# Issuing the last three quad transfers of the down-projection weights earlier in SyncE's queue

## The chip, the cores and the metric

The kernel runs on one core of one Trainium2 chip. The metric is the device time of one execution in microseconds (us). Before the change it is 816.56 us, the median of three runs (816.48 to 816.95).

## What is computed

Three stages follow one another, for a batch of 4 and a sequence of 448 tokens: attention with 12 heads of 64 and a soft cap on the scores, a mixer with a 768x768 theta product, sines and cosines, and a 768x768 channel product, and a second mixer:

```python
def _moe2_ref(x, w_tok1, w_tok2, w_ch1, w_ch2):          # x: (4, 448, 768)
    xt = x.transpose(0, 2, 1)
    h = np.maximum(xt @ w_tok1, 0.0) @ w_tok2            # tokens: 448 -> 256 -> 448
    u = x + h.transpose(0, 2, 1)
    h2 = np.maximum(u @ w_ch1, 0.0) @ w_ch2              # channels: 768 -> 1536 -> 768
    return (u + h2).astype(np.float32)
```

The change touches only the stretch that computes `u @ w_ch1` for the first two of the four batch elements, and in it only the preparation of `w_ch2`.

## The kernel before

All large products are fp32. Each operand is split into a rounded part `hi` (ScalarE, ACT) and a remainder `lo` (VectorE, DVE), and TensorE (PE) makes three matmuls for each pair of tiles (L1716 to L1718: hi by hi, hi by lo, lo by hi).

The two channel products of the second mixer are done in two rounds (s = 0 and 1; two batch elements each) by a seven-product scheme of the Strassen kind on 2x2 blocks. The first product ("rise", `w_ch1`) has 6 groups g of 7 products, always in the order M1, M2, M6, M7, M4, M5, M3. The second ("fall", `w_ch2`) takes the same seven in the same order. Every product of the rise needs one weight part of 128x384 (192 KB); it is 9 matmuls on TensorE, three for each of three column blocks. M1, M2 and M4 use blocks of the weights as they are in memory; M6, M7, M5 and M3 use sums of blocks ("quads"), which are prepared once:

- SyncE (SP) loads four blocks, a quad buffer of 768 KB (`load_fall_quads`, DMA at L640);
- GpSimd (POOL) makes four 128x384 additions in place, one after the other (`sum_fall_quads` over `sum_quads`, L878, L880, L882, L884), each counted in `fall_quad_steps`;
- SP waits for all four and writes the buffer to a scratch in HBM (`store_fall_quads`, wait and DMA at L646 and L647).

There are six such pairs (0 to 5) for `w_ch2`. Pairs 0 to 2 are handled before the stretch of the change; pairs 3, 4 and 5 in it. The buffers are 1, 2 and again 1, so the load of pair 5 waits for the store of pair 3 (L639). Two things need all six stores: ScalarE's `copy_first` of group 5 of the first round (L1029 to L1033), which writes over one of the buffers, and the first load of a summed part in the fall (L654 to L656).

SP is the only issuer of DMAs in this stretch, and its program is one list: a wait in it holds back everything behind it. `load_product` (L621, DMA at L630) loads the weight part of one product into one of 7 slots, after the product that used the slot 7 products earlier was read by TensorE (`part_read`). ScalarE rounds a part (L1021) three products ahead of the one that it is otherwise serving; DVE makes its remainder (L1409) at the same lead; TensorE waits for the remainder (L1941) and starts the product. Both work in program order too:

```python
def rise(s, g, steps):                       # ScalarE, L1119
    for m in steps:
        round_part(part_of(s, g, m) + 3)
```

Below, "M6 of group 4" is the product (0, 4, M6), and its part, load, rounding and remainder go by the same name.

Of the kernel before, what the change touches and what calls it, by code (L numbers as in the profile page):

```python
# [63 lines left out]
M1, M2, M3, M4, M5, M6, M7 = range(1, 8)  # L64
# [33 lines left out]
def fall_quads_use(pair):  # L98

    return ((0, 1), (0, 2), (0, 3), (1, 1), (2, 1), (1, 2))[pair]  # L100
# [33 lines left out]
def mixer_kernel(nc, kq_t, v, cap, w_theta, w_tok_r_t, w_tok_i_t, w_ch, w_tok1, w_tok2,  # L134
# [3 lines left out]
    with ctx:  # L138
# [319 lines left out]
        def after(engine, semaphore, value):  # L458

            if value > 0:  # L460
                engine.wait_ge(semaphore, value)
# [27 lines left out]
        def _(sp):  # L489
# [131 lines left out]
            def load_product(s, g, m):  # L621

                q = part_of(s, g, m)
                after(sp, part_read, last_use(q))
                if m in QUADS:
                    sp.wait_ge(quads_stored, 16 * (g + 1))
                    weights = quad_scratch[g, QUADS[m]]
                else:
                    weights = w_ch1[g, int(m == M4), int(m != M1)]
                sp.dma_start(part_raw[SLOTS[q]][:, :], weights).then_inc(part_loaded[SLOTS[q]], 16)  # L630

            def load_fall_quads(pair):

                e, use = fall_quads_use(pair)
                if pair == 0:
                    sp.wait_ge(tok_split, 2)
                elif pair == 3:
                    sp.wait_ge(tok2_ready, D_TILES * BATCH)
                after(sp, fall_quads_stored[e], 16 * (use - 1))  # L639
                sp.dma_start(fall_quads[e][:, :, :], w_ch2[pair].rearrange("m k p n -> p (m k) n")  # L640
                             ).then_inc(fall_quads_loaded[e], 16)

            def store_fall_quads(pair):

                e = fall_quads_use(pair)[0]
                sp.wait_ge(fall_quad_steps, 4 * (pair + 1))  # L646
                sp.dma_start(fall_quad_scratch[pair].rearrange("q p n -> p q n"), fall_quads[e][:, :, :]  # L647
                             ).then_inc(fall_quads_stored[e], 16)

            def load_fall(s, m, pair, g_half):  # L650

                q, group = fall_part(s, m, pair, g_half), 2 * pair + g_half
                after(sp, part_read, last_use(q))
                if m in QUADS:  # L654
                    for e, uses_of_buffer in enumerate((3, 2, 1)):
                        sp.wait_ge(fall_quads_stored[e], 16 * uses_of_buffer)  # L656
                    weights = fall_quad_scratch[group, QUADS[m]]
                else:
                    weights = w_ch2[group, int(m == M4), int(m != M1)]
                sp.dma_start(part_raw[SLOTS[q]][:, :], weights).then_inc(part_loaded[SLOTS[q]], 16)  # L660
# [3 lines left out]
            def spill(b):  # L664

                sp.wait_ge(u2_made, D_TILES * (b + 1))
                sp.dma_start(spilled_rows[:, :, (b - 2) * SEQ:(b - 1) * SEQ], x_of(b)).then_inc(spilled, 16)
# [55 lines left out]
            def store_quarter(s, m, m_half, n):  # L723

                sp.wait_ge(fall_adds_made, fallen(s, m, D_PAIRS - 1))
                sp.dma_start(out_t[2 * s + n].rearrange("(d p) n -> p d n", p=P)[:, m_half:D_TILES:2, :],
                             x_t[:, 0, m_half:D_TILES:2, n * SEQ:(n + 1) * SEQ]).then_inc(out_stored, 16)
# [16 lines left out]
            def load_first_blocks():  # L744

                sp.wait_ge(spilled, 32)
                sp.wait_ge(part_read, fall_part(0, M1, D_PAIRS - 1, 1) + 1)
                for k in range(K_PAIRS):
                    load_block_tile(0, b12_raw[k], 2 * k, 1)
                for k in range(2):  # L750
                    load_block_tile(0, b22_raw[k], 2 * k + 1, 1)
                load_block(B11, block_raw[B11], 0)

            def load_second_blocks():

                sp.wait_ge(part_read, fall_part(0, M2, D_PAIRS - 1, 1) + 1)
                load_block_tile(1, b22_raw[2], 5, 1)
                for k in range(K_PAIRS):
                    load_block_tile(1, b11_raw[k], 2 * k, 0)
                load_block(B21, block_raw[B21], 0)  # L760

            def reload_x(piece):

                n, d0 = piece // 2, 3 * (piece % 2)
                sp.wait_ge(out_stored, 64)
                sp.dma_start(x_t[:, 0, d0:d0 + 3, n * SEQ:(n + 1) * SEQ],
                             spilled_rows[:, d0:d0 + 3, n * SEQ:(n + 1) * SEQ]).then_inc(x_reloaded, 16)

            for s in range(ROUNDS):
                for g in range(0 if s else 2, C_PAIRS):  # L770
                    for m in M_ORDER:
                        load_product(s, g, m)
                        if (s, g, m) == (0, 2, M2):
                            spill(3)
                        elif (s, g, m) == (0, 2, M4):
                            store_fall_quads(3)
                        elif (s, g, m) == (0, 3, M1):
                            load_fall_quads(4)
                        elif (s, g, m) == (0, 3, M3):
                            store_fall_quads(4)  # L780
                        elif (s, g, m) == (0, 4, M2):
                            load_fall_quads(5)
                        elif (s, g, m) == (0, 5, M1):
                            store_fall_quads(5)
                        if (s, g, m) == (1, 0, M4):
                            store_quarter(0, M5, 1, 1)
                        if (s, g, m) == (1, 1, M2):
                            store_quarter(0, M3, 0, 1)
                    if s == 1 and 1 <= g <= 4:
                        reload_x(g - 1)  # L790
                for m in M_ORDER:
                    for pair in range(D_PAIRS):
                        for g_half in range(2):
                            load_fall(s, m, pair, g_half)
                            if (s, m, pair, g_half) == (0, M6, 1, 0):
                                load_first_blocks()
                            if (s, m, pair, g_half) == (0, M7, 1, 0):
                                load_second_blocks()
                            if (m, pair, g_half) == (M7, 0, 1):
                                store_quarter(s, M2, 0, 0)  # L800
                            if (m, pair, g_half) == (M3, 0, 1):
                                store_quarter(s, M4, 1, 0)
# [1268 lines left out]
```

## Time and profile before

| what | value |
|---|---|
| median of three runs | 816.56 us |
| the profiled execution's own time | 816.48 us |
| its span, first to last instruction | 814.3 us |
| TensorE busy | 805.9 us (99%) |
| VectorE busy | 660.1 us (81%) |
| ScalarE busy | 456.6 us (56%) |
| GpSimd busy | 147.4 us (18%) |
| granted TensorE clock, mean | 1.000 |

Times in the profile count from the span's start. The stretch of the change reaches from about 524 us (M7 of group 2) to about 558 us (M1 of group 5). SPq is the row of SyncE's own DMA issues: its start is when the issue began, so a late start there is a wait in SP's program. A DMA's landing is when the last of its sixteen completions arrived.

### The profile page before, as it was taken

The numbers are of one execution on the slowest core, as the hardware profiler recorded it, in microseconds if no ns is written. First come the engines' busy times: TensorE is split into PE (matmuls) and PEld (weight loads), VectorE is DVE, ScalarE is ACT, GpSimd is POOL, SyncE is SP. The second block draws the span as 40 slices with busy tenths as digits, with TensorE's granted clock in tenths as the row PEclk, the third lists the DMA queues.
The fourth block names the chain that finished last, engine by engine and source line by source line (L and its number), as shares of the span: only waits on it lengthen the run. The fifth ranks groups of instructions, "written<-read, shape, count | busy, mean of one in ns | idle before, by whom it ended". The sixth has DMA issues, their size and how long they took to land.

```text
span 814.3 us, 13137 instructions
## 1 busy us (share of the span) xinstructions
PE 805.9 (99%) x4852; PEld 693.7 (85%) x4852; DVE 660.1 (81%) x1060; ACT 456.6 (56%) x687; POOL 147.4 (18%) x108
## 2 busy tenths in 40 slices
PE   9999999999999999999999999999999999999998
PEld 6555555579999999999999999999998889999997
DVE  5899999989967676866566679887979998789884
ACT  6999999947655454822114116344655645457551
POOL 0254566332000000014442320222000000000000
PEclk9999999999999999999999999999999999999999
DMA  6557765444421221325667655665375455543443
GB/s 175 159 143 171 188 164 134 111 107 106 100 75 43 67 67 49 117 88 178 214 212 253 195 151 185 236 217 178 107 254 164 140 175 175 147 137 109 146 121 127
DMA packets 103295, 119.79 MB, mean 147 GB/s; under 512 B 38880, under 2 KB 100928, under 8 KB 103232
## 3 DMA queue, kind: packets, MB, share of 16 engines
q1 hardware_dynamic: 103008, 118.73, 49.7%
q8 instruction: 39, 0.64, 0.4%
q10 hardware_dynamic: 224, 0.23, 0.1%
q14 instruction: 24, 0.20, 0.1%
HBM read 89.96 MB, written 28.96 MB: 146 GB/s over the span
## 4 chain that ended last, share of the span: by engine, by line
PE 83%; DVE 10%; issue 4%; ACT 2%; DMA 1%; SPq 0%; POOL 0%; DVEq 0%; POOLq 0%; ACTq 0%
PE psum L1718 23%; PE psum L1716 23%; PE psum L1717 23%; PE psum L1772 6%; PE psum L1728 4%; PE psum L1799 2%; DVE part_lo L1409 1%; DVE seven_lo L1459 1%; DVE tile_sums L1186 1%; PE psum L1730 1%; DVE block_lo L1401 1%; ACT ring L919 1%; DMA part_raw<-fall_quad_scratch 1%; PE psum L1807 1%; ACT ring L922 1%
## 5 line engine op out<-in xcount | busy, mean ns | idle before, releaser
L1021 ACT ACTIVATE part_hi<-part_raw 128x384 fp32r<-128x384 f32 x168 | 83.9, 516 | 65.2 <-DMA part_raw<-fall_quad_scratch 35.9
L1409 DVE TENSOR_TENSOR part_lo<-part_raw,part_hi 128x384 fp32r<-128x384 f32 x168 | 96.7, 577 | 22.3 <-ACT part_hi L1021 22.2
L1716 PE MATMUL psum<-seven_hi,part_hi 128*128 128x448 f32 x252 | 91.9, 365 | 1.5 <-DVE seven_lo L1459 0.7
L1716 PE MATMUL psum<-block_hi,part_hi 128*128 128x448 f32 x252 | 91.2, 362 | 0.7 <-DVE part_lo L1409 0.7
L1717 PE MATMUL psum<-block_lo,part_hi 128*128 128x448 f32 x252 | 91.4, 363 | 0.0
L1718 PE MATMUL psum<-seven_hi,part_lo 128*128 128x448 f32 x252 | 91.4, 363 | 0.0
L1718 PE MATMUL psum<-block_hi,part_lo 128*128 128x448 f32 x252 | 91.2, 362 | 0.0
L1717 PE MATMUL psum<-seven_lo,part_hi 128*128 128x448 f32 x252 | 91.2, 362 | 0.0
L1772 PE MATMUL psum<-ring,values 128*32 128x448 f32 x768 | 81.4, 542 | 0.3 <-issue 0.3
L919 ACT ACTIVATE ring<-psum,score_scale 128x1344 f32<-128x1344 f32 (+1 forms) x48 | 75.3, 1568 | 8.7 <-PE psum L1730 5.6
L922 ACT ACTIVATE ring<-ring,cap_col 128x1344 f32<-128x1344 f32 (+1 forms) x48 | 77.2, 1608 | 1.6
L1772 PEld LDWEIGHTS psum<-ring,values 128*32 128x32 f32 x768 | 22.8, 109 | 42.8 <-issue 42.8
L1039 ACT ACTIVATE h_raw<-h_raw 128x448 f32<-128x448 f32 x48 | 27.7, 577 | 56.3 <-DVE h_raw L1421 32.4
L1716 PE MATMUL psum<-theta_hi,x_hi 128*128 128x384 f32 x168 | 56.4, 335 | 0.0
L1717 PE MATMUL psum<-theta_lo,x_hi 128*128 128x384 f32 x168 | 56.1, 334 | 0.0
L1718 PE MATMUL psum<-theta_hi,x_lo 128*128 128x384 f32 x168 | 56.1, 334 | 0.0
L1716 PEld LDWEIGHTS psum<-seven_hi,part_hi 128*128 128x128 f32 x252 | 47.2, 187 | 7.4 <-issue 2.0
L1718 PE MATMUL psum<-u_hi,channel_lo 128*128 128x448 f32 x144 | 52.3, 363 | 0.0
L1718 PE MATMUL psum<-token_hi,z_lo 128*128 128x448 f32 x144 | 52.3, 363 | 0.0
L1717 PE MATMUL psum<-u_lo,channel_hi 128*128 128x448 f32 x144 | 52.2, 362 | 0.0
L1717 PE MATMUL psum<-token_lo,z_hi 128*128 128x448 f32 x144 | 52.2, 362 | 0.0
L1716 PE MATMUL psum<-token_hi,z_hi 128*128 128x448 f32 x144 | 51.8, 360 | 0.0
(184 smaller groups left out, 2165.2 us busy)
## 6 DMA issues: line engine op xcount, KB each, us to landing
part_raw<-moe_w_ch SPq DMA_DIRECT2D x72, 192.0 KB, 2.4
kq_raw<-kq_t SPq DMA_DIRECT2D x47, 224.0 KB, 3.9
part_raw<-quad_scratch SPq DMA_DIRECT2D x48, 192.0 KB, 2.4
part_raw<-fall_quad_scratch SPq DMA_DIRECT2D x48, 192.0 KB, 2.4
values<-v SPq DMA_DIRECT2D x48, 112.0 KB, 3.5
inverse_rows<-inverse_scratch SPq DMA_DIRECT2D x12, 448.0 KB, 6.2
rows_scratch<-turned SPq DMA_DIRECT2D x112, 48.0 KB, 1.7
x_rows<-rows_scratch SPq DMA_DIRECT2D x28, 192.0 KB, 2.4
```

The lines of the kernel that those rows point to most:

```text
L919: act.activation(places, psum[:, first:end, 0:SEQ], ACT.Tanh, scale=score_scale[:, :]).then_inc(tanh_done, 1)
L922: act.activation(places, places, ACT.Exp, scale=cap_col[:, :]).then_inc(probs_ready, 1)
L1021: act.activation(part_hi[SLOTS[q]][:, :], part_raw[SLOTS[q]][:, :], ACT.Copy).then_inc(part_hi_made, 1)
L1039: act.activation(h_raw[tile][:, :], h_raw[tile][:, :], ACT.Relu).then_inc(relu_made, 1)
L1186: dve.tensor_tensor(total, tiles_of_both(pair, A0, B0), tiles_of_both(pair, A1, B1), ALU.add).then_inc(tiles_added, 1)
L1409: dve.tensor_tensor(part_lo[slot][:, :], part_raw[slot][:, :], part_hi[slot][:, :].bitcast(F32), ALU.subtract).then_inc(part_lo_made, 1)
L1716: pe.matmul(out, left[0], right[0], start=start, stop=False)
L1717: pe.matmul(out, left[0], right[1], start=False, stop=False)
L1718: return pe.matmul(out, left[1], right[0], start=False, stop=stop)
L1728: b_mm = pe.matmul(psum[:, b_tile, 0:SEQ], left[s][b_rows, b_keys], right[s][b_rows, queries], start=step == 0, stop=step == 2 and b_tile ...
L1772: mm = pe.matmul(psum[rows, VALUES_BANK, 0:SEQ], own[:, block, 32 * h:32 * h + 32], ring[:, ring_place(pair, tile), :], start=n == 0, stop ...
L1799: mm = pe.matmul(psum[32 * n:32 * n + 32, SUMS_BANK, 0:SEQ], weights[:, :], moving, start=True, stop=True)
```

## The change

SP's list in the first round is rearranged; nothing else is touched, and every DMA and wait is still there once.

| step | before: behind the load of | after: behind the load of |
|---|---|---|
| store of pair 3 | M4, group 2 | M7, group 2 |
| load of pair 4 | M1, group 3 | M3, group 2 |
| store of pair 4 | M3, group 3 | M6, group 3 |
| load of pair 5 | M2, group 4 | M4, group 3 |
| store of pair 5 | M1, group 5 | M2, group 4 |

```diff
                         load_product(s, g, m)
                         if (s, g, m) == (0, 2, M2):
                             spill(3)
-                        elif (s, g, m) == (0, 2, M4):
+                        elif (s, g, m) == (0, 2, M7):
                             store_fall_quads(3)
-                        elif (s, g, m) == (0, 3, M1):
+                        elif (s, g, m) == (0, 2, M3):
                             load_fall_quads(4)
-                        elif (s, g, m) == (0, 3, M3):
+                        elif (s, g, m) == (0, 3, M6):
                             store_fall_quads(4)
+                        elif (s, g, m) == (0, 3, M4):
+                            load_fall_quads(5)
                         elif (s, g, m) == (0, 4, M2):
-                            load_fall_quads(5)
-                        elif (s, g, m) == (0, 5, M1):
                             store_fall_quads(5)
```

## Rows read from the trace of the kernel before

**Rows 1.** The page: busy us of each engine, share of the span, instructions

```profile
PE 805.9 (99%) x4852; PEld 693.7 (85%) x4852; DVE 660.1 (81%) x1060; ACT 456.6 (56%) x687; POOL 147.4 (18%) x108
```

**Rows 2.** Two stretches: us, busy (count) of PE, PEld, DVE, ACT, POOL, clock, DMA

```profile
530.00:543.00 13.00, 13.00 (x67) 12.19 (x66) 11.47 (x20) 6.48 (x14) 4.88 (x4) 1.00 0.58 189
543.00:557.00 14.00, 14.00 (x72) 13.13 (x71) 11.94 (x21) 6.29 (x13) 4.38 (x5) 1.00 0.73 226
```

**Rows 3.** SP's waits for POOL, 515 to 575: total us, times, longest

```profile
SPq L647 <- POOL fall_quads L884: 1.4, 3, 0.6
```

**Rows 4.** SP's issues in order of time: start, us, line, transfer

```profile
526.70 0.37 SPq L647 DMA_DIRECT2D fall_quad_scratch<-fall_quads  x1
...
529.58 0.32 SPq L630 DMA_DIRECT2D part_raw<-quad_scratch  x1
...
531.76 1.69 SPq L640 DMA_DIRECT2D fall_quads<-moe_w_ch  x1
...
543.07 0.37 SPq L647 DMA_DIRECT2D fall_quad_scratch<-fall_quads  x1
...
546.16 0.49 SPq L640 DMA_DIRECT2D fall_quads<-moe_w_ch  x1
...
557.39 0.37 SPq L647 DMA_DIRECT2D fall_quad_scratch<-fall_quads  x1
558.38 0.33 SPq L630 DMA_DIRECT2D part_raw<-moe_w_ch  x1
```

**Rows 5.** Issue to landing, us: issues at 516.03, 516.50, 546.16, 543.07, 557.39, 558.38, 426.03; median

```profile
fall_quads<-moe_w_ch SPq DMA_DIRECT2D x1, 768.0 KB, 5.8
part_raw<-quad_scratch SPq DMA_DIRECT2D x1, 192.0 KB, 5.8
fall_quads<-moe_w_ch SPq DMA_DIRECT2D x1, 768.0 KB, 6.2
fall_quad_scratch<-fall_quads SPq DMA_DIRECT2D x1, 768.0 KB, 4.2
fall_quad_scratch<-fall_quads SPq DMA_DIRECT2D x1, 768.0 KB, 4.1
part_raw<-moe_w_ch SPq DMA_DIRECT2D x1, 192.0 KB, 3.5
fall_quad_scratch<-fall_quads SPq DMA_DIRECT2D x1, 768.0 KB, 8.0
part_raw<-quad_scratch SPq DMA_DIRECT2D x48, 192.0 KB, 2.4
```

**Rows 6.** SP's issues around the one of 426.03

```profile
425.61 0.38 SPq L613 DMA_DIRECT2D quads<-moe_w_ch  x1
...
427.72 3.76 SPq L674 DMA_DIRECT2D block_scratch<-block_turned  x4
```

**Rows 7.** POOL's first addition of pairs 4 and 5; ns min/median/max of all six

```profile
537.89 1.40 POOL L878 TENSOR_TENSOR fall_quads<-fall_quads 128x384 f32<-128x384 f32 x1 [11.21 <-DMA fall_quads<-moe_w_ch]
...
552.42 1.27 POOL L878 TENSOR_TENSOR fall_quads<-fall_quads 128x384 f32<-128x384 f32 x1 [9.38 <-DMA fall_quads<-moe_w_ch]
...
L878 POOL TENSOR_TENSOR fall_quads<-fall_quads x6: 1013/1022/1404, 418.4 to 552.4; 128x384 f32<-128x384 f32 x6
```

**Rows 8.** One part from landing (516.50 + 5.8) to remainder: ACT, then DVE

```profile
522.30 0.53 ACT L1021 ACTIVATE part_hi<-part_raw 128x384 fp32r<-128x384 f32 x1 [2.09 <-DMA part_raw<-quad_scratch]
522.86 0.56 DVE L1409 TENSOR_TENSOR part_lo<-part_raw,part_hi 128x384 fp32r<-128x384 f32 x1 [0.86 <-ACT part_hi L1021]
```

**Rows 9.** First matmuls of M7 and M5 of group 3 and M6 of group 4

```profile
547.38 0.36 PE L1716 MATMUL psum<-block_hi,part_hi 128*128 128x448 f32 x1
550.99 0.36 PE L1716 MATMUL psum<-block_hi,part_hi 128*128 128x448 f32 x1
558.18 0.36 PE L1716 MATMUL psum<-block_hi,part_hi 128*128 128x448 f32 x1
```

**Rows 10.** ScalarE's `copy_first` of group 5, the first to need all six stores

```profile
569.18 0.55 ACT L1032 ACTIVATE h_raw<-psum 128x448 f32<-128x448 f32 x1 [1.95 <-PE psum L1718]
```

## The prediction

> **What bounds the kernel.** I read the engines' shares first, then stretches, then SP's issues, and at last single parts. TensorE is busy for 99% of the span [rows 1], and in the two stretches that hold nearly all of the change it is busy all the time, 13.00 of 13.00 us and 14.00 of 14.00, at a granted clock of 1.00, its level of 2.4 GHz [rows 2]. So no wait of TensorE exists here that an earlier transfer could remove. A product is nine matmuls, and its part's load falls due every 1.8 us: M7 and M5 of group 3 start at 547.38 and 550.99, two products apart, and from M5 to M6 of group 4, four products, it is 7.19 [rows 9].
>
> A part's load waits until TensorE has freed a slot, so the loads go out at the products' pace. For POOL, at the quad stores, SP waits only 1.4 us in three waits [rows 3]: the stores now stand where POOL has just finished; the load of pair 4 is issued at 531.76 and its store at 543.07, 11.3 us later; for pair 5 it is 546.16 and 557.39, 11.2 us [rows 4]. The change shortens the list between load and store: for pair 4 from six part loads (M2 to M3 of group 3) to three (M1, M2, M6), for pair 5 from six to four (M5, M3 of group 3, M1, M2 of group 4). At 1.8 us each that is 5.4 and 7.2 us instead of 10.8, while load, landing and four additions need about 11. The wait at the store must grow, and behind it on SP's queue stand the loads of parts.
>
> **What can be won.** Nothing that I can find. The last store is issued at 557.39 and lands 4.1 us later, at 561.5 [rows 4, 5]. The first instruction that needs it starts at 569.18, and it waited for TensorE [rows 10]. The store is 7.7 us early already. No instruction is removed or added, so the sum has only waits in it.
>
> **Step 1, the store of pair 3.** Before it is issued at 526.70, after a short wait for POOL [rows 3, 4]. It can't go earlier, as its additions are where they were. M4 of group 2, which stood in front of it, now goes behind: 1.1 us later, and landing behind the store. TensorE wants M4 only four products after M1 of that group; ScalarE rounds it after its copy of M1. I cost it at nothing; the cover is the seven slots. Without that cover it would be those 1.1 us.
>
> **Step 2, load and store of pair 4.** The load goes out behind M3 of group 2 (529.58, 0.32) at 529.95, 1.8 us earlier. Loads of this kind take 5.8 and 6.2 us to land [rows 5]; with 6.0 it is 535.95. From POOL's first addition to the store's issue it was 543.07 - 537.89 = 5.18 us for pair 4 and 557.39 - 552.42 = 4.97 for pair 5 [rows 4, 7]; I take 5.05, so the store goes out at 541.0. M6 of group 3, the part in front of it, is issued near 535.0 (1.8 us per part from 529.58). SP then stands for 5.7 us. Queued behind it are M7 (due 536.8), M4 (538.6) and M5 (540.4). An issue takes about 0.4 us with its gap, so M7 goes at 541.4, M4 at 541.8, the load of pair 5 at 542.2, then M5 and M3.
>
> When does M7 land? A part that was issued 0.47 us behind a quad load took 5.8 us: it landed 0.5 us after that load (522.3 against 521.8). One issued 0.99 us behind a store took 3.5: 561.9 against the store's 561.5 [rows 4, 5]. So a small load behind a large transfer lands about 0.45 us after it; the stores took 4.1 and 4.2 [rows 5]: M7 at 541.0 + 4.15 + 0.45 = 545.6. From landing to the remainder it is 522.30 to 523.42, 1.1 us [rows 8]; with 0.1 for TensorE's start, 1.2. M7 is ready at 546.8, and TensorE wants it at 547.38 [rows 9]. It holds by 0.6 us.
>
> Here a rule of the Trainium skill bears, and it speaks against the change. "DMA: Bandwidth & Descriptors", section "Queues, rings and completion order", says that on each DMA engine descriptors are consumed in ring order and that the completion is counted only after all earlier writes of that engine. The two rows on parts behind a large transfer agree. If instead a part landed on its own after 2.4 us, the median of these loads in the profile's page [rows 5], all of the late parts here would be in time and the sum would be nothing.
>
> **Step 3, load and store of pair 5.** Its buffer is free (the store of pair 3 landed near 531). Its load at 542.2 stands behind 768 KB of store and two parts. Alone such loads took 5.8 and 6.2; in the thickest queue of the trace a quad transfer took 8.0 [rows 5]. I take 6.3, nearest to the load of 546.16, which also had a store and parts ahead of it: landing 548.5. M5 of group 3, right behind, lands at 549.0 and is ready at 550.2; TensorE wants it at 550.99 [rows 9]: 0.8 us of spare. POOL needs 5.05 us again: store at 553.55, against 557.39. But M2 of group 4 is in front of it, issued at 545.8: SP stands for 7.4 us. M6 of group 4 was due at 547.6 and now goes at 554.0. It lands behind the store, 553.55 + 4.15 + 0.45 = 558.15, and is ready 1.2 us later, at 559.35. TensorE wants it at 558.18 [rows 9]. **TensorE idles 1.2 us before M6 of group 4.**
>
> The parts behind it land about 0.45 us apart, while TensorE takes 1.8 for each, so no second wait follows. The waits for M7 and M5 of group 3, if they come, don't add to this one: the time of M6 hangs on SP and POOL, not on TensorE. After it every load waits for TensorE's reading again and all of the rest shifts by the same amount, as TensorE is the bound (99%).
>
> **Sum.** The profiled execution took 816.48 us (span 814.3), 0.08 below the median. 816.48 + 1.2 = 817.7; on the median's footing 817.8, or 0.15% more.
>
> **Bounds of the unknown terms.** Short end: loads 5.8 and 5.8, additions 4 x 1.02 us, the median of the first of them [rows 7], and 0.1 between two, 4.4 in all. Then the store of pair 4 goes at 540.15, the load of pair 5 at 541.35, the second store at 551.55; M6 is ready 4.15 + 0.45 + 1.2 = 5.8 us later, at 557.35: no idle time. Long end: additions of 5.2 and a load of pair 5 in 8.0 us: first store at 541.15, load at 542.35, second store at 555.55, M6 ready at 561.35, 3.2 us idle; if the second store took 8.0 us too, 7.0. I take the middle, because the nearest rows in time, kind and queue are those of pairs 4 and 5.
>
> **Rivals.**
> - *The cover just holds* (22%). M6 of group 4 comes within some 0.3 us of its time. For it: the waits of 0.6 and 0.8 us that remain at M7 and M5, and that the additions on POOL are short where DVE is idle. Against: DVE is busy for 11.94 of 14.00 us there [rows 2], and the additions of pairs 4 and 5 began with 1.40 and 1.27 us in place of 1.02 [rows 7]. Time 816.5.
> - *The queue backs up* (27%), the rival on the slower side. Its place is the burst after SP's first stand: store, two parts, load, two parts, 2.3 MB within 2.5 us. Price: each us that the load of pair 5 lands later than 548.5 is one us of idle TensorE; it decides from about 549.0 on, where the total passes 0.2%. For it: the 8.0 us row. Against: that row had another 768 KB right ahead and four more stores behind it [rows 6]. With 8.0 us the idle time is 1.2 + 1.7 = 2.9, 819.5; with M5 and M3 of group 3 late too it is still 2.9.
> - *Faster* (4%): the additions leave the stretch from 552 to 557, and DVE's remainders there run alone. But TensorE waits for none of them [rows 2]. At most some tenths: 816.2.
>
> The forecast itself has 47%, a quarter of it or less (10%) above 1.63 us.
>
> **How the numbers follow.** 0.2% is 1.63 us and about what can be told from no change. Slower: 27 + 10 = 37%. Within 0.2%: 37 + 22 = 59%. Faster: 4%. The range goes from the case without a wait, 816.5, less the run's noise, to somewhat over 3.2 us of idle time (816.56 + 3.2 = 819.8): 816.4 to 819.9. The 7.0 us are outside, as the second store has no large transfer right ahead of it.
>
> **What would show it.** SP's issues: stores of pairs 4 and 5 at about 541.0 and 553.6, SP waiting at L647 for POOL some 5.7 and 7.4 us instead of under 1; M6 of group 4 issued at about 554.0; ScalarE idle before its rounding, ended by a DMA; one gap of TensorE near 558, ended by DVE's L1409. Wrong would be: no gap (then a landing or an addition is shorter than here), a gap at 547 or 551 (then the queue behind the first store is slower), or any gain.

## The result, and the profile after

The changed kernel takes 820.19 us (median of five runs, 818.53 to 822.99) against 816.48 for the kernel before (814.87 to 816.95). The ratio is 1.0057, 95% interval 1.0033 to 1.0082: slower, by 3.7 us. Two later comparisons of the same two kernels gave 819.50 against 816.07 (1.0036, 1.0013 to 1.0059) and 819.77 against 816.54 (1.0039, 1.0019 to 1.0059). The prediction was 817.8, with a range up to 819.9; the first median lies just above that range, the two later ones inside it. The direction and the place were right; the size was not.

The profiled execution took 819.77 us, with a span of 817.6 against 814.3. First the page's shares, then the two stretches of [rows 2] and the one behind them (columns as there):

```profile
PE 806.3 (99%) x4852; PEld 690.0 (84%) x4852; DVE 663.0 (81%) x1060; ACT 456.8 (56%) x687; POOL 145.0 (18%) x108
```

```profile
530.00:543.00 13.00, 13.00 (x67) 12.19 (x66) 12.38 (x20) 6.09 (x13) 4.79 (x4) 1.00 0.54 174
543.00:557.00 14.00, 12.42 (x61) 10.65 (x60) 9.21 (x16) 4.82 (x10) 4.66 (x4) 1.00 0.63 210
557.00:570.00 13.00, 11.83 (x59) 10.78 (x58) 10.45 (x22) 6.66 (x14) 0.00 (x0) 1.00 0.64 200
```

The shares say nothing: TensorE is "99%" busy in both. The stretches do. From 543 to 557 TensorE was busy for 14.00 of 14.00 us and now is for 12.42, and behind 557 it is idle for 1.17 more. Its clock is granted in full (1.00). The cause is one row of SP's waits, 515 to 575, where [rows 3] had 1.4 us:

```profile
SPq L647 <- POOL fall_quads L884: 18.5, 3, 8.4
```

SP's issues, to be read beside [rows 4]: the three quad stores (L647), the two quad loads (L640), and the parts (L630) behind them.

```profile
527.62 0.37 SPq L647 DMA_DIRECT2D fall_quad_scratch<-fall_quads  x1
...
530.24 0.51 SPq L640 DMA_DIRECT2D fall_quads<-moe_w_ch  x1
...
534.88 0.33 SPq L630 DMA_DIRECT2D part_raw<-quad_scratch  x1
542.18 0.38 SPq L647 DMA_DIRECT2D fall_quad_scratch<-fall_quads  x1
542.66 0.44 SPq L630 DMA_DIRECT2D part_raw<-quad_scratch  x1
543.46 0.69 SPq L630 DMA_DIRECT2D part_raw<-moe_w_ch  x1
544.20 0.56 SPq L640 DMA_DIRECT2D fall_quads<-moe_w_ch  x1
...
555.63 0.38 SPq L647 DMA_DIRECT2D fall_quad_scratch<-fall_quads  x1
556.11 1.72 SPq L630 DMA_DIRECT2D part_raw<-quad_scratch  x1
```

M6 of group 3 goes out at 534.88, and then SP issues nothing for 6.9 us, until POOL is done. The store of pair 5 is issued at 555.63, 1.8 us earlier than before, but SP had stood before it for 8.4 us, with M6 of group 4 next in its list. How long the quad loads of 530.24 and 544.20, the store of 555.63 and the part of 556.11 took to land (last number), as in [rows 5]:

```profile
fall_quads<-moe_w_ch SPq DMA_DIRECT2D x1, 768.0 KB, 6.8
fall_quads<-moe_w_ch SPq DMA_DIRECT2D x1, 768.0 KB, 6.4
fall_quad_scratch<-fall_quads SPq DMA_DIRECT2D x1, 768.0 KB, 4.4
part_raw<-quad_scratch SPq DMA_DIRECT2D x1, 192.0 KB, 4.3
```

POOL's first additions, as in [rows 7], then ScalarE's rounding of M7 of group 3 and of M6 of group 4, each ending a wait for a DMA:

```profile
537.12 1.02 POOL L878 TENSOR_TENSOR fall_quads<-fall_quads 128x384 f32<-128x384 f32 x1 [9.53 <-DMA fall_quads<-moe_w_ch]
...
550.71 1.22 POOL L878 TENSOR_TENSOR fall_quads<-fall_quads 128x384 f32<-128x384 f32 x1 [8.56 <-DMA fall_quads<-moe_w_ch]
```

```profile
547.44 0.52 ACT L1021 ACTIVATE part_hi<-part_raw 128x384 fp32r<-128x384 f32 x1 [3.73 <-DMA part_raw<-quad_scratch]
...
560.48 0.52 ACT L1021 ACTIVATE part_hi<-part_raw 128x384 fp32r<-128x384 f32 x1 [2.78 <-DMA part_raw<-quad_scratch]
```

And TensorE's first matmuls of M7, M5 and M3 of group 3 and of M6 of group 4, the answer to [rows 9]; the bracket is the idle time before it and what ended that:

```profile
548.70 0.44 PE L1716 MATMUL psum<-block_hi,part_hi 128*128 128x448 f32 x1 [1.24 <-DVE part_lo L1409]
...
552.50 0.44 PE L1716 MATMUL psum<-block_hi,part_hi 128*128 128x448 f32 x1
...
554.88 0.44 PE L1716 MATMUL psum<-block_hi,part_hi 128*128 128x448 f32 x1 [0.34 <-DVE part_lo L1409]
...
561.74 0.44 PE L1716 MATMUL psum<-block_hi,part_hi 128*128 128x448 f32 x1 [1.17 <-DVE part_lo L1409]
```

Before, these stood at 547.38, 550.99, 552.78 and 558.18. The delay is 1.3, 1.5, 2.1 and 3.6 us: not one gap at the end but a row of them, and the last brings the sum to what SP and POOL dictate. The brackets leave out part of each gap, because a matmul's shown duration (0.36) is longer than its pace (0.20); starts are the better measure.

The gap before M3 is of another kind than the others. Its part had landed at 551.6 (issued at 545.58, 6.0 us), 3.3 us before TensorE started it. It waited for VectorE, which had fallen behind with M7, M4 and M5 and then needed 1.39 us for this remainder, where [rows 8] had 0.56:

```profile
553.34 1.39 DVE L1409 TENSOR_TENSOR part_lo<-part_raw,part_hi 128x384 fp32r<-128x384 f32 x1
```

In the fourteen profiles, 54 remainders between 517 and 571 us took 1.36 to 1.42 us, and every one of them overlaps POOL's additions by 0.95 us or more. The reverse doesn't hold: some remainders took 0.55 us beside an addition. No run takes the additions alone away, so that they are the cause is likely, not shown.

The instruction that needed all six stores [rows 10] came with TensorE as before, later by the same delay:

```profile
572.82 0.55 ACT L1032 ACTIVATE h_raw<-psum 128x448 f32<-128x448 f32 x1 [1.22 <-PE psum L1718]
```

### The profile page after: what moved, and what is told of

Its sections match the earlier page's. It is cut to its first block, busy times and chain, and to the rows that moved or that the text cites. A ratio compares the mean times of both kernels' runs of the same rounds, so it can differ in the third digit from the quotient of the medians.

```text
span 817.6 us, 13137 instructions
## 1 busy us (share of the span) xinstructions
PE 806.3 (99%) x4852; PEld 690.0 (84%) x4852; DVE 663.0 (81%) x1060; ACT 456.8 (56%) x687; POOL 145.0 (18%) x108
## 4 chain that ended last, share of the span: by engine, by line
PE 73%; DVE 16%; issue 4%; DMA 3%; ACT 2%; SPq 1%; POOL 0%; DVEq 0%; POOLq 0%; ACTq 0%
PE psum L1716 20%; PE psum L1718 20%; PE psum L1717 20%; PE psum L1772 6%; PE psum L1728 4%; DVE part_lo L1409 2%; DVE seven_lo L1459 2%; PE psum L1799 2%; DMA part_raw<-quad_scratch 1%; DVE block_lo L1401 1%; DVE tile_sums L1186 1%; ACT ring L919 1%; DMA part_raw<-fall_quad_scratch 1%; PE psum L1730 1%; DVE cos_z L1292 1%
## 5 line engine op out<-in xcount | busy, mean ns | idle before, releaser
L1716 PEld LDWEIGHTS psum<-block_hi,part_hi 128*128 128x128 f32 x252 | 47.3, 188 | 8.3 <-issue 5.3
```

Source lines behind the costliest of these rows:

```text
L1716: pe.matmul(out, left[0], right[0], start=start, stop=False)
```

## The experiments

Below, "delay" is the start of M6 of group 4 on TensorE, less the start of M7 of group 1, less the 36.0 us that lie between them in the kernel before (20 products of 1.8 us). It is blind to what an execution lost earlier. The change's own profile has a delay of 3.65 us. Edits are to SP's list, given against the changed kernel. "Idle time" of TensorE in a profile is the time between the starts on both sides of a gap, less the pace of 0.20. "SP stands" means that it waits at a store (L647) for POOL.

### e1: loads early, stores where they were

```diff
-  (0, 2, M7): store 3     (0, 3, M6): store 4     (0, 4, M2): store 5
+  (0, 2, M4): store 3     (0, 3, M3): store 4     (0, 5, M1): store 5
```

> Loads of pairs 4 and 5 where the change puts them (behind M3 of group 2 and M4 of group 3), all three stores where they were before. My theory (SP stands at a store that waits for POOL, and the part loads queued behind it come late): no stand over 1 us is left at L647, no gap of TensorE near 547 to 562, time as before, 816.5 within 0.5. Rival (the quad loads, moved earlier, crowd the DMA queue and make parts land late): part of the loss stays, 818 or more.

Measured: 815.96 against 816.07, ratio 0.9991 (0.9972 to 1.0009). SP waits once for POOL, 0.8 us; delay 0. So loading early costs nothing. The traffic of the early loads is not the loss.

### e2: pair 5 alone moved

```diff
-  (0, 2, M7): store 3     (0, 2, M3): load 4     (0, 3, M6): store 4
+  (0, 2, M4): store 3     (0, 3, M1): load 4     (0, 3, M3): store 4
```

> Pair 5 moved as in the change (load behind M4 of group 3, store behind M2 of group 4), pairs 3 and 4 left as before. My theory: the load goes out near 538.9, POOL does pair 4 until 543 and pair 5 from about 545.5 to 550.5; SP stands at the store for some 4.4 us, M6 of group 4 lands near 555 and is ready near 556.2, 2 us ahead of its time (558.2): no gap, 816.5 within 0.5. Rival (the position of the last store alone costs it): 818 or more.

Measured: 815.93 against 816.07, ratio 0.9999 (0.9979 to 1.0020). SP stands 3.8 us at the last store (issued at 549.18), and the delay is 0. The last store stands exactly where the change has it and is harmless, because its load went out at 538.5 and not at 544.2. The store of pair 4 goes out on SP's own queue at 542.09, 20.6 us after M7 of group 1 (20.1 in the change), and no product is late: a store at that time does no harm where no part had to wait behind it.

### e3: pairs 3 and 4 alone moved

```diff
-  (0, 3, M4): load 5     (0, 4, M2): store 5
+  (0, 4, M2): load 5     (0, 5, M1): store 5
```

> Pairs 3 and 4 moved as in the change, pair 5 left as before. My theory: SP stands 6 to 7 us at the store of pair 4, M7 of group 3 lands near 547 and TensorE idles there 0 to 1.5 us; the parts behind it have no quad load among them and are in time; M6 of group 4 too. 817.9, between 816.6 and 818.5. Rival (pair 5's second stand is all of the loss, as my forecast had it): 816.5.

Measured: 818.30 against 816.07, ratio 1.0034 (1.0010 to 1.0057); delay 2.07 us. SP stands 6.9 us. SP's burst behind it:

```profile
541.68 0.38 SPq L647 DMA_DIRECT2D fall_quad_scratch<-fall_quads  x1
542.16 0.44 SPq L630 DMA_DIRECT2D part_raw<-quad_scratch  x1
542.96 0.70 SPq L630 DMA_DIRECT2D part_raw<-moe_w_ch  x1
543.76 1.03 SPq L630 DMA_DIRECT2D part_raw<-quad_scratch  x2
544.84 0.96 SPq L630 DMA_DIRECT2D part_raw<-moe_w_ch  x2
```

M7 started 1.2 us late (1.4 in the change's first profile). Another 0.8 us arise before M2 of group 4, whose remainder started late and took 1.37 us beside POOL's additions for pair 5:

```profile
556.35 1.37 DVE L1409 TENSOR_TENSOR part_lo<-part_raw,part_hi 128x384 fp32r<-128x384 f32 x1
```

With this the first stand alone costs over 2 us, where my forecast had it covered.

### e4: the changed kernel again

No edit.

> The changed kernel once more, for a second profile of the same program. My theory: 820.2 between 818 and 825; the sum of TensorE's gaps in 515 to 600 goes with the landing times of the quad loads of pairs 3 to 5 and of the last store. If the spread of 7 us between executions of it came from elsewhere, the profile's gaps there would be the same 3.6 us while its time differs.

Measured: 819.50 against 816.07. This profile took 818.97 us and has a delay of 2.46. Its first store of a stand went out 541.31 - 522.49 = 18.82 us after M7 of group 1 started, against 20.09 in the first profile (542.18 - 522.09): the quad load of pair 4 landed in 5.8 us instead of 6.8. TensorE's gap before M7 of group 3 follows it: 0.1 us here, 1.4 in the first profile, and 2.6 in the third (e12), where that store came after 21.37 us. So the spread of this load goes straight into the gap.

### e5, e6, e7: one stand only, at three places

Pairs 3 and 4 as before; load of pair 5 right behind the store of pair 4; the store of pair 5 at three places.

```diff
-  (0, 2, M7): store 3     (0, 2, M3): load 4     (0, 3, M6): store 4
-  (0, 3, M4): load 5      (0, 4, M2): store 5
+  (0, 2, M4): store 3     (0, 3, M1): load 4     (0, 3, M3): store 4, load 5
+  (0, 4, M2): store 5     # e6: (0, 4, M1), e7: (0, 4, M6)
```

> Pairs 3 and 4 as before; the load of pair 5 right behind the store of pair 4 (behind M3 of group 3), its store behind M2 of group 4 as in the change. So SP has no stand at the store of pair 4 and one at the store of pair 5. My theory: load at 543.5, landing 549.9, store at 554.9, M6 of group 4 ready at 561.1 against 558.2: one gap of 2.9 us, before M6 alone, 819.0 (818.2 to 819.8). Rival (the first stand makes the loss, and the two add up): about 816.1 plus what the change costs beyond pairs 3 and 4 alone, 1.3, that is 817.4.

> As e5, the store of pair 5 one product earlier in the list, behind M1 of group 4. The store's own issue is bound by POOL and stays at 554.9. My theory (the idle time is the time of that store, plus landing and splitting, less the due time of the first part queued behind it): M2 of group 4 is the first, due 1.8 us earlier, so 4.7 us idle, 820.8. Rival (traffic or the store's own time make the loss, not what stands behind it): the same time as e5.

> As e5, the store of pair 5 one product later, behind M6 of group 4. My theory: M7 of group 4 is the first behind it, due 1.8 us later: 1.1 us idle, 817.2. Rival as in e6: the same time as e5.

| store of pair 5 behind | first part behind it | idle expected | idle in the profile | time less before | ratio |
|---|---|---|---|---|---|
| M1, group 4 | M2 | 4.7 | 5.0 | 7.4 | 1.0106 (1.0080 to 1.0131) |
| M2, group 4 | M6 | 2.9 | 3.4 | 5.2 | 1.0074 (1.0054 to 1.0094) |
| M6, group 4 | M7 | 1.1 | 1.2 | 2.4 | 1.0041 (1.0025 to 1.0056) |

The store itself was issued at 554.70, 555.33 and 554.86, at nearly the same time, as its additions dictate. The idle time falls by 1.6 and 2.2 us per product, about the 1.8 of one product. So for these three the rule is: time of the store, plus about 4.9 us to the landing of the part behind it, plus 1.3 to split it, less the due time of that part. The last line's median is 1.2 us above its idle time, while its profiled run (817.82) is 1.3 above the median of before; that leftover I can't attribute.

The first two lose more than they idle, and their times miss what I had expected (820.8 and 819.0; measured 823.99 and 821.71). The reason is a thing I had not priced, the granted clock. (Line numbers of these kernels are one less.) For the store behind M1, TensorE's rows and then its stretches (the clock is the third number from the right):

```profile
555.70 0.37 PE L1717 MATMUL psum<-block_hi,part_lo 128*128 128x448 f32 x1
560.92 0.71 PE L1715 MATMUL psum<-block_hi,part_hi 128*128 128x448 f32 x1 [4.86 <-DVE part_lo L1408]
561.43 0.58 PE L1716 MATMUL psum<-block_lo,part_hi 128*128 128x448 f32 x1
```

```profile
555.00:560.00 5.00, 1.06 (x6) 0.65 (x4) 0.00 (x0) 0.34 (x1) 0.00 (x0) 0.89 0.87 266
560.00:565.00 5.00, 4.08 (x11) 3.71 (x12) 4.18 (x8) 4.30 (x10) 0.00 (x0) 0.50 0.47 167
565.00:570.00 5.00, 5.00 (x24) 4.66 (x24) 3.86 (x8) 1.41 (x3) 0.00 (x0) 0.92 0.30 83
```

After 5.0 us of idling the clock is at 0.50 (1.2 GHz) over the whole stretch from 560 to 565: from 560.92 on, eleven matmuls start in 4.1 us, where the pace of 0.20 gives some 20. By M4 of group 4 the kernel was 7.4 us late, 2.3 more than it had idled; with the store behind M2 it was 5.1, 1.7 more. The medians are 7.4 and 5.2 us above the kernel before; the two profiled executions themselves (823.18 and 821.04) are 6.6 and 4.5 above its median.

### e8: stores where the change has them, loads earlier still

```diff
-  (0, 2, M3): load 4     (0, 3, M4): load 5
+  (0, 2, M1): load 4     (0, 3, M2): load 5
```

> Stores of pairs 3, 4 and 5 exactly where the change puts them, but the loads earlier still: pair 4 behind M1 of group 2, pair 5 behind M2 of group 3. POOL then has finished pair 4 near 531 and pair 5 near 545 when SP comes to their stores. My theory: only the stand at pair 3 stays (1 to 3 us, covered), no gap of TensorE, 816.1 within 0.6. Rival (early stores put their 768 KB ahead of part loads that are due, whether or not SP has to stand): 817.5 or more.

Measured: 817.83 against 816.55, ratio 1.0017 (0.9994 to 1.0040), which can't be told from no change. But the median misses what I had expected (816.1 within 0.6) and lies where the rival had it, and the changed kernel was not measured on this chip beside it. The profiled run was the second fastest of ten: 816.01, with a delay of 0.49. In it SP waits once, 2.5 us, at the store of pair 3; the other two stands are gone with all three stores in place, and M7 of group 3 and M6 of group 4 wait for nothing. The 0.5 us come from elsewhere, before M2 of group 2. Its part had landed at 527.0, 4 us before it was due, though behind an early load of pair 4 that took 7.6 us. But POOL, with pair 4 there so early, added without a pause from 521.9 to 532.1, and three remainders in a row took 1.37 to 1.41 us, that of M2 the last (529.82 to 531.19, due at 530.92). What the slower executions of this kernel lost isn't shown.

### e9: the stores issued by GpSimd

```diff
-  (0, 2, M7): store 3     (0, 3, M6): store 4     (0, 4, M2): store 5     # on SP
+  # on GpSimd, behind the four additions of pairs 3, 4 and 5:
+  pool.wait_ge(fall_quad_steps, 4 * (pair + 1))
+  pool.dma_start(fall_quad_scratch[pair]..., fall_quads[e]...).then_inc(fall_quads_stored[e], 16)
```

> Loads of pairs 4 and 5 where the change puts them; the stores of pairs 3 to 5 are issued by GpSimd itself, right behind its additions, so nothing on SP waits for POOL. Store of pair 4 near 541, as in the change. My theory (the wait on SP's list is the loss): all parts are issued on their beat, no gap of TensorE, 816.3 within 0.6. Rival (768 KB written at 541, among the parts' loads, makes them late by itself): M7 and M4 of group 3 land late, 817.5 or more.

Measured: 816.59 against 816.54, ratio 1.0002 (0.9981 to 1.0022); delay 0. The store of pair 4 in this kernel:

```profile
541.84 0.77 POOL L898 DMA_DIRECT2D fall_quad_scratch<-fall_quads  x1 [0.31 <-POOL fall_quads L878]
```

(Line numbers behind POOL's additions differ in this kernel.) It goes out at 541.84, within half a microsecond of the change's 542.18, and no product waits; SP, which doesn't stand, sends the load of pair 5 at 538.8 instead of 544.20, so POOL is done with that pair earlier too. The 768 KB written at that time don't hurt, here from POOL's queue and in e2 from SP's; SP's wait in front of the parts does.

### e10: only the second stand taken away

```diff
-  (0, 4, M2): store 5
+  (0, 5, M1): store 5
```

> The change with the store of pair 5 put back behind M1 of group 5: only SP's second stand goes. Parts M5, M3 of group 3 and M1 of group 4 still land behind the early load of pair 5. My theory: TensorE idles before M7 and some of the next parts, 1.0 to 2.3 us in all (the delay of M2 of group 4 in the two profiles of the change), so 818 (817.3 to 818.8); the second stand is worth the other 1.3 to 1.5. Rival (as I forecast: the first stand costs nothing): 816.4.

Measured: 817.97 against 816.54, ratio 1.0024 (1.0005 to 1.0042); delay 2.04. On the same chip the change itself was 3.2 above. Its stretches:

```profile
545.00:550.00 5.00, 4.01 (x20) 3.45 (x20) 1.75 (x4) 1.83 (x4) 0.00 (x0) 1.00 1.05 365
550.00:555.00 5.00, 4.67 (x23) 3.81 (x22) 4.39 (x7) 2.41 (x5) 4.62 (x4) 1.00 0.53 172
555.00:560.00 5.00, 5.00 (x26) 4.60 (x26) 5.00 (x10) 2.76 (x6) 0.07 (x1) 1.00 0.42 115
560.00:565.00 5.00, 5.00 (x27) 4.69 (x26) 4.38 (x10) 2.48 (x7) 0.00 (x0) 1.00 0.77 253
```

The idle time near 547 to 555 stays, that behind 560 is gone.

### e11: the first stand one product later

```diff
-  (0, 3, M6): store 4
+  (0, 3, M7): store 4
```

> The change with the store of pair 4 one product later, behind M7 of group 3. M7 is then in time, and M4, due 1.8 us later, is the first behind the store; the load of pair 5 goes out some 0.5 us sooner. My theory (the two stands don't add up: M6 of group 4 hangs on SP's and POOL's chain): the total falls only by those 0.5 us or less, 819.2 (818.6 to 820.0). Rival (they add up): less by the 1.3 us that M7 waits in the change, 818.2 or below.

Measured: 819.14 against 816.54, ratio 1.0032 (1.0015 to 1.0050); delay 3.36. M7 of group 3 was in time and M4 was the first late one. The total fell by 0.6 against the change on the same chip (819.77), less than the 1.3 that M7 no longer waits, but the intervals of the two overlap, so by the times alone this isn't settled. The profile says more: M6 of group 4 comes 6.2 us after the store's issue (555.33 to 561.52), as it does in the change (6.1, 6.2 and 6.1 in its three profiles), whatever was idle before. The load of pair 5 was not 0.5 us sooner, as I had expected, but went out 22.1 us after M7 of group 1, as in the change: the store before it came 0.9 us later, as pair 3's load had been slow (7.0 us).

### e12: the changed kernel a third time

No edit.

> The changed kernel on the same chip as e10 and e11, to compare with them. Both theories: about 3.3 to 3.7 us above the kernel before, 819.8 within 1.0.

Measured: 819.77 against 816.54. The profiled run was the slowest of the twelve, 823.06 us, with a delay of 4.88; another 1.7 us were lost before M7 of group 1. The kernel before has slow executions too (up to 821.48 on this chip). Two of TensorE's rows, and its stretch:

```profile
548.94 0.37 PE L1718 MATMUL psum<-block_hi,part_lo 128*128 128x448 f32 x1
551.78 0.71 PE L1716 MATMUL psum<-block_hi,part_hi 128*128 128x448 f32 x1 [2.48 <-DVE part_lo L1409]
```

```profile
550.00:555.00 5.00, 3.22 (x9) 2.90 (x10) 2.72 (x5) 2.82 (x6) 1.43 (x1) 0.66 0.91 338
```

Both quad loads were slow (6.9 and 7.1 us), the gap before M7 of group 3 grew to 2.6 us, and then the clock was granted at 0.66 on average: M7's nine matmuls reached from 551.78 to 555.13, 3.35 us instead of 1.8. So in this execution the changed kernel paid for the clock too.

## Why the prediction was wrong, and where it was right

**Right: the mechanism.** Nothing could be won, as TensorE never waited there; the waits at the stores grow (forecast 5.7 and 7.4 us, in the first profile 6.9 and 8.4); the parts queued behind them come late; the loss goes into M6 of group 4 and stays. Taking the wait off SP's list (e9), or leaving pairs 3 and 4 where they were and loading pair 5 early (e2), brings the time back. Loading pairs 4 and 5 earlier still (e8) takes both stands out of the profile, though its median leaves this open. And moving what stands behind the wait moves the loss by a product's time (e5 to e7). That the two stands don't add up held too, as far as e11 can tell.

**Step 1** made no product late by itself, as forecast. But it pushed M5 and M3 of group 2 and with them the load of pair 4, from 529.95 to 530.24, and where pair 3's load was slow (7.0 and 6.9 us in e11 and e12) to 531.3 on the time scale of the kernel before. So the store of pair 3 is a third wait in the same chain, which I had priced at nothing.

**Wrong: step 2, "It holds by 0.6 us"** for M7 of group 3. It came 1.3 us late in the first profile, and e3 and e10 show that the first stand alone costs 1.4 to 2.2 us. Two terms failed. The first is the landing of the part behind the store, 4.15 + 0.45 us: M7's part landed 5.3 us after the store's issue (542.66 + 4.8, against 542.18), and from that issue to M7 on TensorE it was 6.4 to 6.5 us in all five profiles with this stand (the change's three, e3 and e10), where I had 5.8. That alone uses up the 0.6 us: in e4 the store went out just when I had forecast it, 18.8 us after M7 of group 1, and M7 of group 3 was still 0.1 us late. The second is the quad load's landing (6.0 us). Over the fourteen profiles, that of pair 3, whose place no kernel changes, took 5.7 to 7.0 us, and that of pair 4 5.8, 6.8 and 7.1 in the three profiles of the change. I read two rows and took their mean as if it were fixed; even the long end of my bounds kept it. And the waits behind M7 weren't all for DMAs: I had priced every remainder at 0.56 us, and those beside POOL's additions took up to 1.4.

**Wrong: step 3, the size, in "An issue takes about 0.4 us with its gap".** From the store of pair 4 to the load of pair 5 I had 1.2 us; it was 2.0, since the starts behind the first part lie 0.7 to 0.8 us apart when SP sends this burst (542.66, 543.46, 544.20); what slows them isn't shown. The terms, forecast and measured in the change's first profile:

| term | forecast | measured |
|---|---|---|
| store of pair 4 issued | 541.0 | 542.18 |
| to the load of pair 5 | 1.2 | 2.02 |
| landing of that load | 6.3 | 6.4 |
| POOL's four additions, to the store | 5.05 | 5.0 |
| store to landing of the part behind it | 4.6 | 4.8 |
| splitting it, and TensorE's start | 1.2 | 1.3 |
| M6 of group 4 starts | 559.35 | 561.74 |

2.4 us too early in all: 1.2 by the first store, 0.8 by the burst, 0.3 by the last store and its part. With 3.6 instead of 1.2 us of idle time the sum would have been 820.1 against 819.77 measured. The burst was even named, as the rival "the queue backs up", but priced by the landing alone; in fact the load landed as forecast and SP's own issues were slow.

**Wrong: the chances.** 59% stood for no measurable change, because each margin of some tenths was counted as kept. But a chain of six serial terms in front of an engine that is busy all the time has no slack to average over: the idle time is the larger of zero and their sum, and a late term is not made good by anything behind it. A version faster than both kernels did not come out of this: e1, e2 and e9 can't be told from the kernel before.

**Not foreseen: the clock.** I took a gap of TensorE to cost its own length. That held for the gaps of up to 1.4 us here (granted clock 1.00 in the first two profiles of the change), and not for those of 2.6 us (e12), 3.4 (e5) and 5.0 (e6).

The rule of the Trainium skill on ring order ("DMA: Bandwidth & Descriptors", "Queues, rings and completion order") agrees with the traces: the parts behind the stores of 542.18 and 555.63 landed 0.8 and 0.4 us after them, not 2.4 us after their own issue. But e9 shows that it wasn't what decides. Parts that were issued before a store land in time beside it.

## What to carry to other kernels

On a queue of one list, a transfer may be issued early at little cost (none in e1, up to 0.5 us in the profile of e8), but a wait may not: put a semaphore wait where its condition is already true, and count what stands behind it. Before moving a wait forward, compare the time from load to store with the work that must fit between them; here it was 11 us, and the list left 5.4 and 7.2. When the producer's end can't be moved, give the wait to the engine that produces.

## What the hardware showed that I had not expected

- In an otherwise full TensorE, a gap of 2.6 us was followed by a granted clock of 0.66 over 5 us (e12), and one of 5.0 us by 0.50 (e6); gaps of 1.2 to 1.4 us left it at 1.00.
- In the burst behind a 768 KB store, SP's first part followed after 0.5 us and the next issues after 0.7 to 0.8 us each, against 0.5 behind a 768 KB load in the kernel before (516.03, 516.50, in [rows 5]).
- VectorE's subtraction for a part (128x384) took 0.55 us, or 1.36 to 1.42 us beside GpSimd's additions.
- The same 768 KB load, at the same place of the same program text, landed in 5.7 to 7.0 us from profile to profile.
